# Opening attention with a third buffer for rows and hats, other groups of tiles, 32-column state sums, and scans ahead of masks

## The reference

```
scale = min(|a|, 0.999) / (|a| + 1e-6);  a = (a_re + i a_im) * scale       # per step and channel
S_t = a_t * S_(t-1) + k_t v_t^T          # complex 48 x 48 state per head; k v real
y_t = q_t . Re(S_t)
x   = y laid out as batch x 768 x 384
h   = relu(x^T @ w_tok1) @ w_tok2;  u = x + h^T                # mixing over time, 768 -> 256 -> 768
x2  = u + relu(u @ w_ch1) @ w_ch2                              # 384 -> 1536 -> 384
out = x2 + relu(layernorm(x2) * g @ w2_ch1) @ w2_ch2           # 384 -> 1536 -> 384
```

## Time and profile before

| what | value |
|---|---|
| time, median of 3 (lowest to highest) | 917.45 us (915.28 to 918.37) |
| the profiled execution's own time | 917.37 us |
| its span in the profile | 915.6 us |
| PE busy, share of the span | 846.4 us, 92% |
| DVE, ACT, POOL busy | 475.3, 415.0, 26.1 us |
| mean granted clock of PE | 0.983 of full |
| last outputs of tile 5 end (the opening's end) | 120.15 us |

### The profile page before, as it was taken

How to read it: one execution, slowest core, us unless ns; L and a number is a source line. 1 busy time by engine, 2 the same in 40 slices (tenths; PEclk the granted TensorE clock), 3 DMA queues, 4 the chain that set the end, 5 groups by cost and what they waited for, 6 DMA issues and landing times. The chain is left out here.

```text
span 915.6 us, 15179 instructions
## 1 busy us (share of the span) xinstructions
PE 846.4 (92%) x6280; PEld 822.7 (90%) x6280; DVE 475.3 (52%) x821; ACT 415.0 (45%) x767; POOL 26.1 (3%) x39
## 2 busy tenths in 40 slices
PE   0757888999999999999999999999999999999998
PEld 0546777999999999999999999999999999999997
DVE  5875568877757775676673454253223313322121
ACT  6766358777727767657663332232112211211111
POOL 1010000000000000000000000000000000000000
PEclk9977899999999999999999999999999999999999
DMA  9935964444524555516342610000001002000000
GB/s 369 178 64 89 240 167 77 81 78 118 101 68 78 103 96 142 105 25 128 65 88 36 232 53 1 1 1 1 26 26 53 27 1 78 1 27 27 1 26 26
DMA packets 46839, 71.07 MB, mean 78 GB/s; under 512 B 5040, under 2 KB 38064, under 8 KB 46256
## 3 DMA queue, kind: packets, MB, share of 16 engines
q1 hardware_dynamic: 46768, 70.09, 32.6%
HBM read 42.86 MB, written 8.26 MB: 56 GB/s over the span
## 5 line engine op out<-in xcount | busy, mean ns | idle before, releaser
L701 ACT ACTIVATE hidden<-bank 128x384 fp32r<-128x384 f32 x192 | 93.7, 488 | 325.1 <-PE bank L333 324.7
L1015 DVE SCALAR_TENSOR_TENSOR hidden<-bank,hidden 128x384 fp32r<-128x384 f32 x192 | 105.8, 551 | 258.3 <-ACT hidden L701 258.3
L331 PE MATMUL bank<-ch,hidden 128*128 128x384 f32 x576 | 192.7, 335 | 3.7 <-DVE x_u L1023 3.6
L333 PE MATMUL bank<-ch,hidden 128*128 128x384 f32 x576 | 192.8, 335 | 0.0
L332 PE MATMUL bank<-ch,hidden 128*128 128x384 f32 x576 | 192.4, 334 | 0.0
L331 PEld LDWEIGHTS bank<-ch,hidden 128*128 128x128 f32 x576 | 108.1, 188 | 4.9 <-issue 4.8
L332 PEld LDWEIGHTS bank<-ch,hidden 128*128 128x128 f32 x576 | 108.1, 188 | 0.0
L333 PEld LDWEIGHTS bank<-ch,hidden 128*128 128x128 f32 x576 | 108.1, 188 | 0.0
L331 PE MATMUL bank<-turned_x,ch 128*128 128x384 f32 x288 | 102.9, 357 | 1.7 <-DVE turned_x L1097 1.7
L332 PE MATMUL bank<-turned_x,ch 128*128 128x384 f32 x288 | 97.1, 337 | 0.0
L333 PE MATMUL bank<-turned_x,ch 128*128 128x384 f32 x288 | 97.0, 337 | 0.0
(11 more groups left out here) (168 smaller groups left out, 1468.6 us busy)
## 6 DMA issues: line engine op xcount, KB each, us to landing
rows<-hats SPq DMA_DIRECT2D x126, 128.5 KB, 4.7
a_t<-in_a_rows_dram SPq DMA_DIRECT2D x20, 384.0 KB, 5.5
qk_t<-in_qk_rows_dram SPq DMA_DIRECT2D x19, 384.0 KB, 5.7
v_t<-in_v_cols_dram SPq DMA_DIRECT2D x24, 192.0 KB, 5.5
plain_ch<-in_moe_w_ch_dram SPq DMA_DIRECT2D x6, 768.0 KB, 10.6
out_dram<-x_u SPq DMA_DIRECT2D x24, 192.0 KB, 2.0
x_kept_dram<-x_u SPq DMA_DIRECT2D x18, 192.0 KB, 3.8
x_u<-x_kept_dram SPq DMA_DIRECT2D x18, 192.0 KB, 3.1
```

Of the source, the lines that this page charges most:

```text
L331: nc.tensor.matmul(ps, lhs_h, rhs_h, start=first, stop=False, skip_group_check=True)
L333: return nc.tensor.matmul(ps, lhs_l, rhs_h, start=False, stop=final, skip_group_check=True)
L701: nc.scalar.activation(hid_h[:, m % NHID, :], hid_ps[m % 2][:, 0:HALF], ACT.Relu).then_inc(hidden_rounded, 1)
L1015: nc.vector.scalar_tensor_tensor(out=hid_l[:, m % NHID, :], in0=hid_ps[m % 2][:, 0:HALF], scalar=0.0, in1=hid_h[:, m % NHID, :].bitcast(F3 ...
```

## The change

Four things are changed; the arithmetic is the same. **(1) Buffers:** in the opening rows and hats get a third buffer each (rows in the unused second half of `x_u`, hats in raw room of the channel weights), tile n uses buffer n % 3. **(2) Order of the opening:** ACT and DVE prepare unit 1 alone, then units 2 and 3 together, then unit 4; `keep_khat(1,0)` comes ahead of `sines(1)`; rounding of piece 0 is moved from after `round_turns(1)` to ahead of `round_turns(0)`; ACT takes three looks and DVE one; SP's issues are reordered; the dummy matmuls after tiles 0 to 5 number 2, 22, 4, 16, 2, 0. **(3) `chunk_state`** uses three groups of 32 stationary columns where it had one of 96. **(4) In a slot of the weave** `turn_scan` of the next tile stands ahead of `mask(n, 0)` (not in slot 6), `add_u` ahead of `mask(n, 1)` in slot 3 of a batch, and `row_stats`, `rest_x` and `round_x` later; in slot 6 ACT's `keep_khat(6,1)` comes ahead of the table change.

```diff
-    SUMMED = 2
+    SUMMED = 3
+        hats_early = [hats] + [room.rearrange(...) for room in hats_room]      # three
+        rows_early = [rows[:, 0, :, :], rows[:, 1, :, :], x_u[0:D2, 1, 0:H * (2 * P + 1)].rearrange(...)]
         def hats_before(n):
-            return n - 2 if n <= NT else n - 1
+            return n - 3 if n <= NT else n - 1
+        def rows_slot(n):
+            return n % 3 if n < NT else n % 2
+        def rows_before(n):
+            return max((i for i in range(n) if rows_slot(i) == rows_slot(n)), default=None)
         # lay_rows (SP)
-                if n > 1:
-                    sp.wait_ge(outputs_ready, 2 * (n - 1))
-                    sp.wait_ge(states_decayed, links(n - 1))
+                before = rows_before(n)
+                if before is not None:
+                    sp.wait_ge(outputs_ready, 2 * (before + 1))
+                    sp.wait_ge(states_decayed, links(before + 1))
         # SP, weights of the channel layer
             for n in WEIGHTS[2:2 + PER_MLP]:
+                if n == 2 + THIRDS:
+                    wait_rows(sp, NT - 1)
                 load_piece(n)
         # ACT, slot n == NT
-                    use_turns()
+                    keep_khat(n, 1)
+                    use_turns()
         # ACT, start
             look(1)
+            round_piece(act, 0)
             for part in (round_turns, sines, decays):
                 part(0)
             use_logs()
-            for u in (1, 2):
-                square(u)
-                inverse_of_re(u)
-            log_magnitude(1)
+            for part in (square, inverse_of_re, log_magnitude):
+                part(1)
+            look(2)
             keep_khat(0, 0)
-            log_magnitude(2)
+            growth(1)
             keep_khat(0, 1)
         # ACT, rest (its beginning)
                 round_turns(1)
-                round_piece(act, 0)
+                keep_khat(1, 0)
                 sines(1)
-                keep_khat(1, 0)
                 decays(1)
                 keep_khat(1, 1)
-                round_turns(2)
-                round_piece(act, 1)
+                use_logs()
+                for u in (2, 3):
+                    square(u)
+                for u in (2, 3):
+                    inverse_of_re(u)
                 keep_x(1, slow)
                 round_x(1)
+                log_magnitude(2)
+                log_magnitude(3)
+                keep_khat(2, 0)
+                growth(2)
+                keep_khat(2, 1)
+                growth(3)
+                use_turns()
+                angle(2)
+                angle(3)
         # DVE, slot
-                mask(n, 0)
                 if n == NT:
+                    mask(n, 0)
                     step(0)
...
                     prepare(n + 1, turn_scan)
+                    mask(n, 0)
                     step(0)
+                    prepare(n + 1, turns_wrapped)
                     if j == ST:
-                        for i in range(0, ST, 2):
-                            rest_x(b * NT + i)
+                        add_u(2 * (b - 1))
                     mask(n, 1)
         # PE, chunk_state
-                    last = nc.tensor.matmul(m_ps[0:D2, h * D:(h + 1) * D], khat[:, h * D2:(h + 1) * D2], v_head(n, h), start=True, stop=True)
+                    for lo in range(0, D2, GROUP):
+                        last = nc.tensor.matmul(m_ps[lo:lo + GROUP, h * D:(h + 1) * D], khat[:, h * D2 + lo:h * D2 + lo + GROUP], v_head(n, h),
+                                                start=True, stop=True)
         # PE, opening
-                for i in range(6):
+                for i in range((2, 22, 4, 16, 2, 0)[n]):
                     keep_busy()
```

More of the change, by code:

```diff
@@ L36, in gated_scan_mixer_mlp_kernel @@
     SC = 4
+    GROUP = P // 4
     NHID = 3
@@ L706, in slot @@
                 keep_khat(n, 0)
+                if n == NT:
+                    round_piece(act, 5)
+                    growth(n + 1 - PAIRS)
+                    keep_khat(n, 1)
+                    use_turns()
+                    angle(n + 1 - PAIRS)
+                    step(1)
+                    prepare(n + 1, round_turns, sines)
+                else:
+                    prepare(n + 1, round_turns)
+                    step(1)
+                    prepare(n + 1, sines)
+                    keep_khat(n, 1)
+                prepare(n + 1, decays)
+                step(2)
+                use_logs()
+                prepare(n + 2, square, inverse_of_re, log_magnitude)
                 if j == ST:
@@ L1107, in _ @@
                 part(0)
-            abs2(1)
-            least(1)
-            for part in (ratio0, ratio_step):
+            for part in (abs2, ratio0, ratio_step, log_sums):
                 part(1)
-            abs2(2)
+            mask(0, 0)
             dve.wait_ge(minima_done, LOOKS - SUMMED)
@@ L1118, in _ @@
             nc.vector.reduce_sum(bad[:, 0:1], step_low[:, :], axis=AX.X).then_inc(flag_counted, 1)
-            mask(0, 0)
-            for part in (ratio0, ratio_step):
-                part(2)
+            rest_piece(dve, 0)
             mask(0, 1)
-            log_sums(1)
-            log_sums(2)
             dve.wait_ge(flag_summed, 1)
             nc.vector.tensor_copy(flag[:, :], banks[1][0:1, 0:1]).then_inc(flag_set, 1)
+            turn_scan(1)
             add_state(0)
-            turn_scan(1)
             dve.wait_ge(flag_set, 1)
@@ L1133, in _ @@
             rest_x(0)
+            mask(1, 0)
             turns_wrapped(1)
-            turn_scan(2)
-            rest_piece(dve, 0)
-            mask(1, 0)
             grown_qk(1)
@@ L1140, in _ @@
             turn_hats(1)
-            turns_wrapped(2)
+            abs2(2)
+            abs2(3)
+            ratio0(2)
+            ratio_step(2)
             add_state(1)
             rest_x(1)
-            grown_qk(2)
-            abs2(3)
             ratio0(3)
             ratio_step(3)
+            log_sums(2)
             mask(2, 0)
-            turn_hats(2)
-            mask(2, 1)
+            log_sums(3)
+            mask(2, 1)
+            grown_qk(2)
+            turn_scan(2)
+            grown_qk(3)
+            turns_wrapped(2)
+            add_state(2)
+            turn_scan(3)
+            turn_hats(2)
+            rest_x(2)
+            mask(3, 0)
+            turns_wrapped(3)
+            mask(3, 1)
+            turn_hats(3)
+            rest_piece(dve, 1)
+            add_state(3)
+            rest_x(3)
             abs2(4)
@@ L1153, in _ @@
             ratio_step(4)
-            log_sums(3)
             log_sums(4)
-            add_state(2)
-            rest_x(2)
-            mask(3, 0)
-            turn_scan(3)
-            mask(3, 1)
-            turns_wrapped(3)
-            grown_qk(3)
-            add_state(3)
-            turn_hats(3)
-            rest_x(3)
-            turn_scan(4)
-            rest_piece(dve, 1)
             mask(4, 0)
-            turns_wrapped(4)
             mask(4, 1)
             grown_qk(4)
+            turn_scan(4)
             add_state(4)
+            turns_wrapped(4)
             rest_x(4)
@@ L1254, in scores @@
                 for g in range(HB):
-                    last = nc.tensor.matmul(scored[:, g * P:(g + 1) * P], rows[:, n % 2, part * HB + g, P:2 * P],
-                                            rows[:, n % 2, part * HB + g, 0:P], start=True, stop=True)
+                    last = nc.tensor.matmul(scored[:, g * P:(g + 1) * P], rows_of(n)[:, part * HB + g, P:2 * P],
+                                            rows_of(n)[:, part * HB + g, 0:P], start=True, stop=True)
                 last.then_inc(scores_ready, 1)
```

114 lines of the change are left out of this document (50 added, 64 removed).

## The result

The changed kernel takes 902.77 us (median of 4 runs, 899.38 to 903.52), the kernel before 917.08 (4 runs, 915.28 to 918.37) beside it: ratio 0.9838 [0.9808, 0.9869], 14.3 us faster. The forecast was 900, its range 890 to 910.

The account below looks back on a forecast made before the run. The opening was taken as one chain through ACT and DVE, the weave and tail as bound by PE. From 917.37 us, -16 (opening) -3.6 (`add_u`) +0.4 (slot 6) +1.7 (state sums) = -17.5 gave 899.9, said as 900; range 890 to 910.

Parts of the forecast that it names:

- The start: Start of the opening: 2.8 us later, through DVE's look at the fourth load and ACT's rounding of piece 0.
- The opening, -16: Opening, through tile 5: 16 us faster, from the reordered ACT and DVE lists, later start included.
- The walk through the lists: Opening: new ACT and DVE lists timed with old durations; put `mask(5,1)` at 100.1, 17.3 us earlier.
- rival A: Opening gives only what unit 1 alone gives, for 908.7 us in total; chance 0.14.
- all handoffs together: Opening: some fifteen handoffs between 41 and 100 us, at 0.1 us each, were put at 1.3 us.
- Here the third buffer pays: Opening, tile 4: rows no longer wait for tile 2's state; removes a plain wait of 9 us, issue at 76.8.
- unit 1's 7.2: Opening: preparing unit 1 alone brings its hats 7.2 us earlier, `turn_hats(1)` at 54.0 instead of 61.20.
- Slot 6, +0.4: Weave, slot 6: moving `keep_khat(6,1)` removes PE's 1.6 us wait, but tile 7's rows wait grows to 4.9; 0.4 lost.
- `add_u`, -3.6: Weave: `add_u` ahead of `mask(n,1)` removes PE's wait of 1.2 us in each of three batches, 3.6 in all.
- State sums, +1.7: Weave: 32-column sums at 29 ns a record plus another grouping change cost 0.11 us a tile, 1.7 lost.
- Rival B: State sums overlap better, 18 ns a record, gaining 0.4 us a tile, 6 in all; total 892; chance 0.14.
- the forecast's own signs of being wrong: Tile 2's transposes later than 68, `mask(5,1)` later than 106, or `chunk_state` taking 2 us or 1.

Follow-up runs that it names:

- e3: The changed kernel without the flag's load and the branch on ACT and DVE (slow path left out): 897.08 us, ratio 0.9806.
- e5: The kernel before without the flag's load and the branch on ACT and DVE (slow path left out): 917.18 us, ratio 1.001.
- e10: The changed kernel with the flag made 15 us earlier, ahead of the first hats, and the branch kept where it is: 900.47 us, ratio 0.9828.
- e7: The changed kernel with 28 more dummy matmuls in waits of the opening, branch left in: 897.31 us, ratio 0.9796.
- e8: The changed kernel with two buffers again for rows and hats in the opening: 903.85 us, ratio 0.9848.
- e9: The changed kernel with `add_u` and `row_stats` back behind `mask(n,1)` and the hidden part: 907.39 us, ratio 0.9894.
- e1: The kernel before with only the state sums changed, to three groups of 32 columns: 911.72 us, ratio 0.9961.
- e6: The changed kernel with `grown_qk` of the next tile ahead of `mask(n,1)` in the weave's slots, except slot 6: 898.79 us, ratio 0.981.
- e2: The changed kernel with the state sums back in one group of 96 columns: 903.68 us, ratio 0.9866.
- e11: The changed kernel with early flag, late `mix_down` in the opening, early `grown_qk` in the weave and more dummies in the opening: 892.10 us, ratio 0.9743.
- e12: As e11, but with the state sums in one group of 96 columns: 900.25 us, ratio 0.9832.
- e4: The changed kernel with `mix_down` of the last tile behind outputs and `chunk_state` in the opening: 899.84 us, ratio 0.9815.

## Why the prediction came out right

**The start.** `round_turns(0)` 26.42 (forecast 25.9), first hats 30.96 (30.5): right to half a microsecond, both by way of the fourth load and piece 0.

**The opening, -16: this step failed, and got 6.7.** By its marks:

| mark | forecast | after | late by | new in it |
|---|---|---|---|---|
| `angle(1)` | 44.9 | 45.26 | 0.4 | |
| `turn_hats(1)` | 54.0 | 57.51 | 3.5 | ACT's 5.3 at the branch |
| `turn_k(2,0)` | 64.4 | 68.10 | 3.7 | |
| `turn_hats(3)` | 81.0 | 86.06 | 5.1 | 4.5 of it gone in e3 |
| end of `add_state(4)` | 95.6 | 106.47 | 10.9 | outputs and `mix_down`, half clock |
| `mask(5,1)` | 100.1 | 111.20 | 11.1 | |

The walk through the lists gave each instruction the later of its engine's end and its producer's end, but only for ACT and DVE. It missed two things. An instruction with no row in the trace, the load of the flag and the branch, was free before because ACT had work queued, and unit 1 alone took that work away (e3, e5, e10). With the branch out, and the clock full from 40 to 60 us, 6.8 of the 11.1 at `mask(5,1)` are gone. And PE was taken as instant: behind `mask(n,1)` come six matmuls of `mix_down`, 64 of outputs and the sums, some 4.7 us at mostly half clock from `mask(3,1)` (85.45) to the end of tile 3's outputs (90.2). At full clock and with the stall as it is, `mask(5,1)` stands 5.9 earlier (e7). The forecast did name the clock, as a reason for rival A, and then put only 1.3 us on all handoffs together (its own fifteen at 0.1 make 1.5; no row shows the 0.1). The handoff from `mask(4,1)` to `add_state(4)` alone took 5.1.

"Here the third buffer pays" was wrong. The plain wait of 9 us was real, but in the new lists the hats of tile 4 are made at 80.34 and laid at 81.37, and with two buffers at 81.70 (e8): once DVE makes them behind tile 2's masks, the buffer is free by itself. So the third buffer did not remove the wait, and that the new order did is read from these rows. No run undoes the regrouping, the earlier `keep_khat(1,0)`, the move of piece 0 or the dummies one by one, so how the 6.7 divide between them is open. Rival A's argument against itself rested on this step.

Rival A (908.7) was right on the opening, 6.7 against its 7.2, though not by its reason alone: unit 1's 7.2 arrived only as 3.7 at `turn_hats(1)` (61.20 to 57.51), and more came later.

**Slot 6, +0.4: right in size by coincidence.** The wait for k-hat went and the one for tile 7's rows grew from 2.91 to 3.81, not to 4.9; the other part is a wait of 2.00 that the forecast did not have, for DVE's remainder of a hidden value (`rest_hidden`, L1045) in this slot.

**`add_u`, -3.6: right.** The wait disappeared, returned alone when it was undone (e9), and is worth 4.6 there, a little more than its waits.

**State sums, +1.7: mis-sized and with the wrong sign.** A record takes 17 ns and not 29, 0.81 us in place of 1.38, 0.57 saved a tile. Rival B (18 ns) had the mechanism; its 6 us did not show in the total either, because two stretches gave it back: about half in the chain of rows (e1, e6), and, less surely, the opening, where the changed kernel's granted clock is lower than e2's and T6 3.6 later. So the step that failed here is the time of a record, taken from the 64-column rows. The drain at a change of column grouping that the Trainium skill names ("TensorEngine Tiling (Array Packing)", Key Properties) does not make 32 columns a loss: from the last output to the sums the distance is 0.21 us (290.86 to 291.07), as before 0.22. The least distance of about 25 ns that the Trainium skill gives ("TensorE: Matmul & The Clock Gate", part "Wait - 56ns, not 53.3ns?") is undercut by the measured 17 ns of the three groups.

So the total came from a sum with two wrong terms: 9.3 less in the opening, 6.2 more in the weave. Its direction was earned, its number was luck: all three of the forecast's own signs of being wrong came true, tile 2's transposes later than 68 (68.10), `mask(5,1)` later than 106 (111.20) and `chunk_state` at 1 us or under (0.81).

## What to carry to other kernels

Before shortening a chain, list the instructions that have no row in the trace (register loads, branches) and ask which queued work hid them; they reappear when that work goes. In a stretch that is one chain, walk all engines' queues, PE's at the clock that its own waiting will get it, and don't credit a buffer for a wait that the new order removes. When the bounding engine's work shrinks, look for the next chain in the same slot: here the sums' 3.7 us became 8.15 once the chain of rows and the clock were seen to.

## What was not expected of the hardware

- The state sum's 48 records with stationary parts of 32 columns in three groups start every 17 ns; 64 columns in two groups every 29 ns, 96 in one every 85 ns.
- The load of a register and the branch hold ACT for 4.8 us with its operand ready 15 us before (e10; 4.7 in e11 and e12), and 5.0 to 5.5 in the kernels with the later flag (e2, e4, e6 to e9), yet in the kernel before it was over within 3.4 us of the flag (46.5 to 49.92) and under other work. Which part of it takes the time is open. The DMA share from 40 to 60 us was 0.41 there and 0.56 after. Packets of the DMA queue of instructions, q14, lie at 48.0, 50.0 and 52.5 us in the kernel before and at 49.0, 49.5 and 51.5 in the changed one, to half a microsecond; without the branch there is one (e3) or none (e5) from 40 to 54. A wait for instructions behind other transfers would fit; it was not tried.
- The granted clock of the same opening differs between executions: in the mix stretch's window, 115 to 130 us, it was 0.77 in the changed kernel, 0.90 in e6 and 0.89 in e9. In the changed kernel the mix ran at half clock (1.2 GHz) from 117.3 to 123.3 us and took 13.64 us; it took 12.98 with 96-column sums at full clock (2.4 GHz, e2), but also 13.00 with 32-column sums at full clock in e4. So the pair of the changed kernel and e2 does not show that shorter sums lower the clock. That dummies raise it is shown by e7.
